# Two MLP layers in transposed tiles: the widths of the last two token pairs change places

## The chip, the cores and the metric

The kernel runs on one core of one Trainium2 chip. The metric is the device time of one execution in microseconds (us); lower is better. The kernel before takes 1495.45 us, the median of three runs (1495.42 to 1497.24).

## The reference

Attention without softmax (squared ReLU of the scores), then two MLP layers over the same 6016 tokens, all in float32:

```
scores = matmul(z, z.T) / S              # z: 2 x 3008 x 64
x = u * matmul(maximum(scores, 0)**2, v) # u, v: 2 x 3008 x 256
h = x @ w_in;  x = (h - tanh(h)) @ w_out             # 256 -> 2048 -> 256
x = (sigmoid(x @ w_gate) * (x @ w_val)) @ w_out2     # 256 -> 1536 -> 256
```

## The kernel before

Everything is kept transposed: features lie on the 128 partitions and tokens along the free dimension. A float32 product is made of three matmuls (L523 to L525, L630 to L635): each operand is cut in a high part that the fast float format holds (written by ScalarE) and the rest (written by VectorE), and high times high, high times low and low times high are summed in PSUM.

The attention comes first (to about 480 us) and isn't touched. Then come the two MLP layers. Each works on six *pairs* of token tiles; `PAIR_WIDTHS` (L65) holds the tokens of one tile of each pair, and `pair_width(q)` and `pair_token(q)` give the width and the first token of pair q. Pairs 0 to 5 belong to the first MLP, pairs 6 to 11 to the second, with the same six widths. A pair is worked through in *units* of two blocks of hidden features: 8 units in the first MLP, 6 in the second.

For a unit n TensorE makes the first products of a 2x2 block scheme with seven products in place of eight (`product`, L619): seven products of three matmuls in the first MLP (21), twice that in the second (42, for gate and value). They go to PSUM tile `hidden`. ScalarE and VectorE take them out (`snapshot`, L870 to L875; `combine`, L1136), apply tanh or sigmoid, subtract or multiply, and split the result in `part_hi` (ScalarE, `high`, L882) and `part_lo` (VectorE, `low`, at L1046, a helper that all splits share). With these the second products (`second`, L699 to L716) add 24 matmuls a unit to PSUM tile `acc`. The order of TensorE's work is written out by hand (L785 to L799): the first products of unit n alternate with the second products of unit n - 1. A pair has therefore 8 x (21 + 24) = 360 matmuls in the first MLP and 6 x (42 + 24) = 396 in the second. Each matmul loads its own 128 x 128 weights, in the instruction before it (engine PEld in the rows).

At the change of pairs the two widths mix for one unit: the first products have the new width, the second products still the old one. In unit 0 of a pair ScalarE writes the finished `acc` of the pair before to `x_out` (`evacuate`, L910 to L916), two tiles in one instruction for each half; in the first MLP the last of these instructions stands in unit 1 (L978 and L979). The first `second` call of the new pair waits for it:

```
                pe.wait_ge(s_lo, half_done(n, b))
                if u == 0 and b < 2:
                    ...
                        pe.wait_ge(s_evac, 2 * q - b)
```

Also during a pair, the next pair's tokens are loaded (`load_x`, L436, on SyncE's queue), combined (`sum_x`, L1094 to L1108) and split (`split_x`, L855 and L1046). `x_out` is stored by SyncE's queue (`store_pair`, L464). The last pair ends by itself: `last_highs` and `last_lows` (L723 to L737), then three evacuations and three stores of one tile and half each (L1034 to L1040, L1294, L513 to L516).

Of the kernel before, what the change touches and what calls it, by code (L numbers as in the profile page):

```python
# [61 lines left out]
    return T // TPB * SEQ + T % TPB * TOK  # L62


PAIR_WIDTHS = (512, 512, 512, 512, 496, 464)  # L65
assert len(PAIR_WIDTHS) == PAIRS and 2 * sum(PAIR_WIDTHS) == ALL and max(PAIR_WIDTHS) <= TOK


def pair_width(q):
    return PAIR_WIDTHS[q % PAIRS]  # L70


def pair_token(q):
    return 2 * sum(PAIR_WIDTHS[:q % PAIRS])

# [1263 lines left out]
```

## Time and profile before

| What | Value |
|---|---|
| median of three runs | 1495.45 us (1495.42 to 1497.24) |
| the profiled execution | 1496.93 us |
| its span, first to last instruction | 1495.1 us |
| TensorE busy | 1489.9 us, 8796 matmuls |
| weight loads (PEld) busy | 1256.0 us |
| VectorE busy | 1135.4 us |
| ScalarE busy | 949.5 us |
| DMA | 241.79 MB, mean 162 GB/s |

A matmul's busy time here is about 0.37 to 0.39 us, but the next one starts some 0.21 to 0.23 us after it: they are pipelined. So neither "busy" nor the mean duration of a matmul is its price; the price is the distance between the starts of two neighbours, which is read from the timeline or from the number of matmuls in a stretch of known length.

### The profile page before, as it was taken

To read this page: it belongs to the slowest core of one execution; us is meant where nothing else is said; L and a number is where in the kernel's file an instruction comes from. 1 tells how busy PE (TensorE), PEld (TensorE's weight loads), DVE (VectorE), ACT (ScalarE), POOL (GpSimd) and SP (SyncE) were. 2 spreads that over 40 slices of the span, in tenths; PEclk is the share of its full clock that TensorE was granted. 3 is DMA by queue.
4 is the path that set the end of the run, shared out by engine and by line. 5 is a ranking of instruction groups with operands and counts; after the bars stand their busy time and mean duration, and the time that the engine had idled before them with its cause. 6 is when DMAs were issued, how large, how long until landed. Compare 5 with 4: busy or idle time off the path is not lost.

```text
span 1495.1 us, 21893 instructions
## 1 busy us (share of the span) xinstructions
PE 1489.9 (100%) x8796; PEld 1256.0 (84%) x8796; DVE 1135.4 (76%) x1416; ACT 949.5 (64%) x1285; POOL 0.5 (0%) x5
## 2 busy tenths in 40 slices
PE   9999999999999999999999999999999999999999
PEld 8888888888888888888888888888888888888888
DVE  8999988999987787777676777666666676666656
ACT  8677767777766666666666666655556555555554
POOL 0000000000000000000000000000000000000000
PEclk9999999999999999999999999999999999999999
DMA  4444422254434345453535456453636454554452
GB/s 141 139 162 151 152 81 86 89 213 159 159 121 172 116 154 186 155 196 131 211 138 186 155 177 234 172 191 127 246 127 218 156 199 173 190 186 185 151 194 89
DMA packets 37365, 241.79 MB, mean 162 GB/s; under 512 B 3600, under 2 KB 8720, under 8 KB 23952
## 3 DMA queue, kind: packets, MB, share of 16 engines
q1 hardware_dynamic: 37120, 240.16, 44.1%
q8 instruction: 69, 1.13, 0.3%
q14 instruction: 32, 0.26, 0.1%
q10 hardware_dynamic: 144, 0.24, 0.0%
HBM read 196.21 MB, written 44.17 MB: 161 GB/s over the span
## 4 chain that ended last, share of the span: by engine, by line
PE 100%; ACT 0%; DVE 0%; issue 0%; DVEq 0%
PE acc L563 25%; PE hidden L632 13%; PE hidden L635 13%; PE hidden L630 13%; PE acc L524 10%; PE acc L525 10%; PE acc L523 10%; PE hidden L550 6%; PE acc L729 0%; PE acc L743 0%; PE acc L736 0%; DVE x_out L1294 0%; ACT part_hi L935 0%; ACT h L932 0%; DVE part_lo L1165 0%
## 5 line engine op out<-in xcount | busy, mean ns | idle before, releaser
L1046 DVE TENSOR_TENSOR part_lo<-h,part_hi 128x1024 fp32r<-128x1024 f32 (+5 forms) x317 | 375.2, 1184 | 82.3 <-ACT part_hi L882 49.9
L874 ACT ACTIVATE snap<-hidden 128x512 f32<-128x512 f32 (+2 forms) x360 | 211.8, 588 | 249.3 <-PE hidden L635 249.0
L632 PE MATMUL hidden<-region 128*128 128x512 f32 (+2 forms) x840 | 323.6, 385 | 0.0
L630 PE MATMUL hidden<-region 128*128 128x512 f32 (+2 forms) x840 | 323.6, 385 | 0.0
L635 PE MATMUL hidden<-region 128*128 128x512 f32 (+2 forms) x840 | 323.5, 385 | 0.0
L563 PE MATMUL acc<-part_hi,region 64*128 64x512 f32 (+1 forms) x2256 | 286.1, 383 | 0.7 <-ACT part_hi L935 0.7
L1136 DVE TENSOR_TENSOR h<-hidden,snap 128x512 f32<-128x512 f32 (+2 forms) x252 | 170.7, 678 | 142.5 <-ACT snap L874 115.7
L525 PE MATMUL acc<-part_hi,region 128*128 128x512 f32 (+2 forms) x664 | 256.1, 386 | 0.0
L524 PE MATMUL acc<-part_lo,region 128*128 128x512 f32 (+2 forms) x664 | 256.0, 386 | 0.0
L523 PE MATMUL acc<-part_hi,region 128*128 128x512 f32 (+2 forms) x664 | 255.9, 385 | 0.0
L563 PEld LDWEIGHTS acc<-part_hi,region 64*128 64x128 f32 x2256 | 216.1, 184 | 39.4 <-issue 1.1
L953 ACT ACTIVATE part_hi<-h 128x1024 fp32r<-128x1024 f32 (+1 forms) x143 | 149.3, 1044 | 129.8 <-PE acc L563 129.0
L882 ACT ACTIVATE part_hi<-h 128x1024 fp32r<-128x1024 f32 (+2 forms) x164 | 170.7, 1041 | 79.9 <-DVE h L1274 42.5
L630 PEld LDWEIGHTS hidden<-region 128*128 128x128 f32 x840 | 157.7, 188 | 30.5 <-issue 0.3
L632 PEld LDWEIGHTS hidden<-region 128*128 128x128 f32 x840 | 157.7, 188 | 29.4
L635 PEld LDWEIGHTS hidden<-region 128*128 128x128 f32 x840 | 157.7, 188 | 29.3
L1188 DVE TENSOR_TENSOR h<-h 128x1024 f32<-128x1024 f32 (+1 forms) x143 | 170.9, 1195 | 0.0
L563 PE MATMUL acc<-part_lo,region 64*128 64x512 f32 (+1 forms) x1128 | 156.4, 383 | 0.0
L523 PEld LDWEIGHTS acc<-part_hi,region 128*128 128x128 f32 x664 | 124.6, 188 | 23.8
L524 PEld LDWEIGHTS acc<-part_lo,region 128*128 128x128 f32 x664 | 124.7, 188 | 23.4
L525 PEld LDWEIGHTS acc<-part_hi,region 128*128 128x128 f32 x664 | 124.7, 188 | 23.4
L941 ACT ACTIVATE h<-hidden 128x1024 f32<-128x1024 f32 (+1 forms) x143 | 142.0, 993 | 0.8 <-PE hidden L550 0.2
(68 smaller groups left out, 1149.9 us busy)
## 6 DMA issues: line engine op xcount, KB each, us to landing
region<-ready SPq DMA_DIRECT2D x33, 2304.0 KB, 8.8
region<-ready SPq DMA_DIRECT2D x51, 1408.0 KB, 6.1
ready<-region SPq DMA_DIRECT2D x6, 2304.0 KB, 7.4
ready<-region SPq DMA_DIRECT2D x8, 1408.0 KB, 6.0
xs<-x_out SPq DMA_DIRECT2D x18, 512.0 KB, 6.0
x_in<-xs SPq DMA_DIRECT2D x16, 512.0 KB, 8.1
snap<-vP SPq DMA_DIRECT2D x24, 256.0 KB, 2.7
u_in<-uT SPq DMA_DIRECT2D x10, 512.0 KB, 5.2
```

The lines of the kernel that those rows point to most:

```text
L523: pe.matmul(dst, w_hi, x_hi, start=start, stop=False, skip_group_check=True)
L524: pe.matmul(dst, w_hi, x_lo, start=False, stop=False, skip_group_check=True)
L525: return pe.matmul(dst, w_lo, x_hi, start=False, stop=stop, skip_group_check=True)
L563: last = pe.matmul(acc[:, 2 * r + d, 0:w], v[ROWS[r], 2 * p + c, half], a[ROWS[r], 2 * (s % 2) + c, 0:w], start=start, stop=False, skip_gr ...
L630: pe.matmul(dst, weights[0], x[0], start=i < 3, stop=False, skip_group_check=True)
L632: pe.matmul(dst, weights[0], x[1], start=False, stop=False, skip_group_check=True)
L635: pe.matmul(dst, weights[1], x[0], start=False, stop=True, skip_group_check=True).then_inc(s_prod[group_of(n, s) % 2], 1)
L874: act.activation(snap[:, g % 2, i, 0:w], hidden[:, CHAIN[g % 2], 0:w], ACT.Copy).then_inc(s_snap, 1)
L882: act.activation(part_hi[:, b, 0:w], h[:, n % 2, b, 0:w], ACT.Copy).then_inc(s_hi, 1)
L1046: return ve.tensor_tensor(dst, whole, hi.bitcast(F32), ALU.subtract)
L1136: ve.tensor_tensor(dst, hidden[:, (BANK2, BANK7, BANK7)[i], 0:w], snap[:, g % 2, (0, 2, 1)[i], 0:w], ALU.add).then_inc(s_add, 1)
L1188: ve.tensor_tensor(full[:, k, :, 0:w], first[:, k, :, 0:w], first[:, k, :, 0:w], ALU.mult).then_inc(s_full, 1)
```

## The change

The last two entries of `PAIR_WIDTHS` change places. Pair 4 of the first MLP and pair 10, its counterpart in the second, hold 464 tokens a tile in place of 496; pairs 5 and 11 hold 496 in place of 464. The number of instructions, their order and the number of columns in all stay the same; the pairs' first tokens, their loads and their stores follow from the widths.

```diff
-PAIR_WIDTHS = (512, 512, 512, 512, 496, 464)
+PAIR_WIDTHS = (512, 512, 512, 512, 464, 496)
```

## Rows read from the trace of the kernel before

**Rows 1.** The page, parts 1 and 2: busy time by engine, TensorE's granted clock.

```profile
PE 1489.9 (100%) x8796; PEld 1256.0 (84%) x8796; DVE 1135.4 (76%) x1416; ACT 949.5 (64%) x1285; POOL 0.5 (0%) x5
PEclk9999999999999999999999999999999999999999
```

**Rows 2.** Stretches of one width, TensorE: us, busy (matmuls), clock, DMA share, GB/s.

```profile
820.00:880.00 60.00, 60.00 (x270) 1.00 0.41 147
1340.00:1400.00 60.00, 60.00 (x274) 1.00 0.43 163
1425.00:1485.00 60.00, 60.00 (x289) 1.00 0.36 135
1000.00:1060.00 60.00, 60.00 (x267) 1.00 0.46 176
```

**Rows 3.** Timeline of TensorE, pair 4 after its unit 0: start, us, engine, line.

```profile
819.74 0.39 PE L523 MATMUL acc<-part_hi,region 128*128 128x496 f32 x1
...
821.08 0.39 PE L523 MATMUL acc<-part_hi,region 128*128 128x496 f32 x1
```

**Rows 4.** The same, in pair 10.

```profile
1343.76 0.38 PE L524 MATMUL acc<-part_lo,region 128*128 128x496 f32 x1
...
1345.08 0.38 PE L632 MATMUL hidden<-region 128*128 128x496 f32 x1
```

**Rows 5.** The same, where pair 4 comes to its first `second` call.

```profile
814.14 0.39 PE L635 MATMUL hidden<-region 128*128 128x496 f32 x1
814.37 0.39 PE L523 MATMUL acc<-part_hi,region 128*128 128x496 f32 x1
```

**Rows 6.** The weight loads there.

```profile
813.93 0.19 PEld L635 LDWEIGHTS hidden<-region 128*128 128x128 f32 x1
814.20 0.19 PEld L523 LDWEIGHTS acc<-part_hi,region 128*128 128x128 f32 x1
```

**Rows 7.** ScalarE's evacuation that this call waits for, in pair 4 and pair 5.

```profile
813.07 1.02 ACT L915 ACTIVATE x_out<-acc 128x1024 f32<-128x1024 f32 x1
...
893.09 0.99 ACT L915 ACTIVATE x_out<-acc 128x992 f32<-128x992 f32 x1
```

**Rows 8.** Timeline, change from pair 10 to 11: 496 between 464, early and late.

```profile
1406.12 0.38 PE L523 MATMUL acc<-part_hi,region 128*128 128x496 f32 x1
...
1407.44 0.37 PE L630 MATMUL hidden<-region 128*128 128x464 f32 x1
...
1413.18 0.38 PE L523 MATMUL acc<-part_hi,region 128*128 128x496 f32 x1
...
1414.52 0.38 PE L630 MATMUL hidden<-region 128*128 128x464 f32 x1
```

**Rows 9.** Timeline, change from pair 5 to 6: 464 between 512.

```profile
960.38 0.37 PE L523 MATMUL acc<-part_hi,region 128*128 128x464 f32 x1
...
961.64 0.39 PE L630 MATMUL hidden<-region 128*128 128x512 f32 x1
```

**Rows 10.** VectorE's split of the next pair's tokens in pair 5: min/median/max ns.

```profile
L1046 DVE TENSOR_TENSOR region<-x_in,region x7: 682/682/682, 921.3 to 949.5; 128x512 fp32r<-128x512 f32 x7
```

**Rows 11.** Timeline of the tail.

```profile
1490.92 0.19 PEld L736 LDWEIGHTS acc<-part_lo,region 128*128 128x128 f32 x1
...
1491.51 0.37 PE L736 MATMUL acc<-part_lo,region 128*128 128x464 f32 x1
1491.99 0.64 DVE L1294 COPY x_out<-acc 128x464 f32<-128x464 f32 x1 [1.11 <-PE acc L736]
1492.65 0.33 SPq L516 DMA_DIRECT2D yT<-x_out  x1
```

**Rows 12.** Groups by shape: VectorE's combine at 496 and at 464.

```profile
L1136 DVE TENSOR_TENSOR h<-hidden,snap 128x496 f32<-128x496 f32 x42 | 28.2, 672 | 24.8 <-ACT snap L874 20.4 <-PE hidden L635 4.4
L1136 DVE TENSOR_TENSOR h<-hidden,snap 128x464 f32<-128x464 f32 x42 | 26.8, 638 | 26.3 <-ACT snap L874 21.9 <-PE hidden L635 4.4
```

**Rows 13.** DMA issues: one of the last stores, KB, median us to landing.

```profile
yT<-x_out SPq DMA_DIRECT2D x3, 232.0 KB, 2.1
```

## The prediction, made before the changed kernel was run

> **What bounds the kernel now.** I read the page first. TensorE is busy for 1489.9 of 1495.1 us at the full granted clock of 2.4 GHz in every slice, and no other engine is over 76% [rows 1]. The chain of waits shows the same: it runs through TensorE's lines for 100% of the span. The list of waits has ScalarE waiting for TensorE and VectorE for ScalarE, and next to nothing the other way. So the time is a sum of distances between the starts of neighbouring matmuls, and I looked at that distance for each width. A 60 us window also counts the one or two matmuls that were still running at its start (one lasts some 0.38 us), so 60 us hold about 1.7 fewer starts than the count. The stretch at 512 tokens then gives 60 / 265.3 = 226 ns, the one at 464 gives 60 / 287.3 = 209 ns. The two stretches at 496 tokens differ: pair 4 gives 60 / 268.3 = 223.6 ns, pair 10 gives 60 / 272.3 = 220.3 ns [rows 2]. The timeline gives it exactly: six starts take 1.34 us in pair 4, which is 223.3 ns each [rows 3], and 1.32 us in pair 10, which is 220.0 ns each [rows 4]. The same shape, the same weights' size, the same clock, and yet two rhythms, 3.3 ns apart, each held for its whole pair. I call 220.0 ns the even rhythm and 223.3 ns the uneven one.
>
> **Where the uneven rhythm starts.** Pair 4 began in the even rhythm too. At its first second product a matmul follows 0.23 us after its neighbour in place of 0.22 [rows 5], and its weight load starts 814.20 - 813.93 = 0.27 us after the load before it in place of 0.22 [rows 6]. It had to wait for the evacuation of pair 3, which ends at 813.07 + 1.02 = 814.09 us [rows 7]. The direct loss is 10 to 20 ns. But from there on the pair stays at 223.3 ns to its end: 60 us later it's still there [rows 2, 3]. I found no place where a run of 496-wide matmuls went back to the even rhythm by itself.
>
> **What the change adds and removes on TensorE.** The matmuls are the same 8796 and the columns are the same in sum: 360 matmuls of each width in the first MLP and 396 of each in the second. If each width has one price, the change is worth nothing there. So the question is the rhythm in which the 496-wide matmuls run once they come after 464-wide ones rather than 512-wide ones. The trace shows this at the change from pair 10 to pair 11, where 464 and 496 alternate for a unit. The first block of six at 496 takes 1407.44 - 1406.12 = 1.32 us, the even rhythm. A few microseconds later such a block takes 1414.52 - 1413.18 = 1.34 us, the uneven one [rows 8]. Nothing else changed but that more 464-wide matmuls had run. A 464-wide matmul takes 209 ns where columns alone would scale 220.0 by 464/496 to 206, and its weight load takes 0.19 us: it runs close to the load, with less room to bring a shifted load back. My reading is that the 464-wide stretch leaves the loads shifted, and that the 496-wide pair takes this over.
>
> - First MLP: pair 5 is the 496-wide one after the change. Of the 360 before, 33 ran at 220.0 (those ahead of the wait at 814.1: 21 in the mixed unit and 12 behind it) and the rest at 223.3. After: all 360 at 223.3. That is 33 x 3.3 ns = +0.11 us.
> - Second MLP: pair 11 is the 496-wide one. Before, 378 of the 396 ran at 220.0 (all but three blocks of six late in the mixed unit, of which [rows 8] show one). After: all at 223.3, +378 x 3.3 ns = +1.25 us. If the even rhythm holds instead, this term is 0; that is its lower bound.
> - 464-wide matmuls, now after 512-wide ones: a block of six between 512-wide ones takes 961.64 - 960.38 = 1.26 us, 210 ns each [rows 9], and a long stretch 209 [rows 2]. I take 209 as before: 0. From below: 206 by columns would give back 756 x 3 ns = 2.3 us, which no row shows for any block. From above: 212, if 464 had an uneven rhythm of its own, +2.3 us; no row shows that for a long stretch either.
>
> **Covers that could be gone.** In pairs 4 and 10 the evacuation of the pair before is 1024 elements wide beside 464-wide matmuls; the nearest row is pair 5's with 992 elements, 0.99 against 1.02 us [rows 7]. The wait at L709 could be 0.03 us longer, once in each MLP: 0 to +0.1 us, I take 0. In pairs 4 and 10 units of 464 carry the loading, combining and splitting of 496-wide tokens. Pair 5 carried 512-wide ones beside 464 without moving TensorE from 209 ns: seven splits of 682 ns [rows 2, 10]. So that costs 0. The x loads and the weights' loads keep their place in SyncE's queue; in pairs 4 and 10 their units are shorter by 5%, as they were in pairs 5 and 11, with DMA busy for 0.36 to 0.48 of the time [rows 2]: 0.
>
> **The tail.** What follows the last matmul is now for 496 tokens. VectorE's copy of 0.64 us [rows 11] grows by the step between 464 and 496 of such an operation, 672 - 638 = 0.03 us [rows 12]; the last matmul's own end by 32 columns, 0.01 us; the last store of 232 KB takes 2.1 us to land [rows 13] and grows to 248 KB: between 0 and 2.1 x 16/232 = 0.14 us. I take +0.1 us in all, bounds 0.04 to 0.2. The last unit's chain (VectorE's product, ScalarE's high part, VectorE's low part) reaches TensorE just in time: its weight load of L736 starts at 1490.92 [rows 11], about when it would anyway. After the change this chain's four operations grow by some 0.03 us each, 0.12, and the 22 matmuls beside it by 11 to 14 ns each, 0.24 to 0.31 us. TensorE stays the later one, and the cover gets better.
>
> **The sum.** 0.11 + 1.25 + 0 + 0.1 = +1.46 us. On the profiled execution, 1496.93 us (span 1495.1 us and 1.8 around it), this gives 1498.4. The median of the runs, 1495.45, is 1.5 us below the profiled execution; on it the sum gives 1496.9. The three runs themselves lie at 1495.42, 1495.45 and 1497.24. It may be that pair 4 wasn't in the uneven rhythm in the two shorter ones; 327 matmuls x 3.3 ns are 1.1 us. No profile of them shows it.
>
> The Trainium skill speaks against this forecast. Its page "TensorE: Matmul & The Clock Gate", section "Back-to-back issue gap", gives the distance of two matmuls as N / 2.4 GHz + 2.5 ns when warm, for the matmul alone, and says that in a stream with weight loads both set it. By the formula alone the price depends on N only, 209.2 ns at 496, and the swap would be worth nothing on TensorE. The rows agree with its slope between 512 and even 496 (226 to 220.0 ns, 16 columns), and with neither its constant nor the second price at 496; the measured distances decide.
>
> **The rivals.**
> 1. *Price by width alone.* The 496-wide matmuls of pair 11 keep 220.0 ns, because it was the late evacuation and not the neighbourhood that shifted them, and 512 or the wait of a new pair sets the rhythm back. For it: pair 4's shift did begin at a wait [rows 5, 6]. After the change the evacuation in pair 11 is narrower and early. Against it: the 1.34 us block in [rows 8], with no such wait in its unit's first half. Then only the tail and the small term of the first MLP are left, +0.1 to +0.2: 1495.6.
> 2. *Both pairs even.* As rival 1, and pair 5 is even too: 327 x 3.3 ns = 1.08 us are gained, less 0.1 for the tail: 1494.5. Against it: in the first MLP the evacuation ends later in the unit than in the second, and the pair begins in 464's rhythm.
> 3. *The timed runs before had both 496 pairs even,* and after both are uneven: 756 x 3.3 ns + 0.1 = +2.6: 1498.0. For it: the 1.8 us between the timed runs; against it: the profile.
> 4. *Slower beyond the measurement.* The 464-wide pairs enter straight from 512 and lock into an uneven rhythm of their own, at 212 ns in place of 209. The place is the first unit of pairs 4 and 10; it decides once their long stretches are above 211 ns. The price is 756 x 3.3 ns = 2.5 us on top of the 1.46: +4.0, 1499.4. For it: a single 464-wide block between 512-wide ones was already at 210 [rows 9]. Against it: the long 464 stretches of both MLPs, entered from two different rhythms, settled at the same 209 ns.
>
> **How the numbers follow.** The forecast (both 496 pairs uneven) 0.55, rival 1 0.17, rival 2 0.06, rival 3 0.12, rival 4 0.05, anything else 0.05. The range holds the forecast, rivals 1 and 3, and their bounds of a few tenths: 1495.0 to 1498.5. About 0.2% (3.0 us) is what a measurement of this kernel can tell from no change. The forecast and rivals 1 and 2 lie within it, rival 3 nearly at its edge at 1498.4, rival 4 beyond. Slower by over 0.2%: rival 4, a quarter of rival 3 and of the rest, 0.09. Faster by over 0.2% needs 3 us less of a gapless TensorE: 0.01. Same: 0.90.
>
> **What would show it.** In the trace of after, pair 11's long stretch at 496: six starts in 1.34 us (forecast) or 1.32 (rival 1). Pair 5's: the same question (rival 2). The long 464 stretches at 209 (or 212, rival 4), TensorE without a gap at L709, and from the last L736 matmul to the end of the span about 3.7 us, where before has 1495.1 - 1491.5 = 3.6 [rows 11]. The prediction is wrong if a 496-wide pair after a 464-wide one runs evenly, or if the two rhythms turn out to be set by something that differs from one execution to the next.

## The result

The changed kernel takes 1498.45 us (median of 19 runs, 1497.63 to 1499.01). The kernel before, on the same chip, takes 1495.42 us (19 runs, 1494.64 to 1497.37). The medians lie 3.0 us apart; the ratio is 1.0018 with a 95% interval of 1.0012 to 1.0024, which is 1.8 to 3.6 us. That is clear of the noise, and it lies on the 0.2% (3.0 us) that the prediction drew as its line for "same", which the interval spans. The prediction was +1.5 us, 1496.9, with a range up to 1498.5: the measured change is twice the forecast one, and the time lies 0.05 us inside the range.

The profiled execution of after took 1497.91 us, its span is 1496.1 us. The page, parts 1 and 2, beside [rows 1]:

```profile
PE 1490.8 (100%) x8796; PEld 1270.6 (85%) x8796; DVE 1135.4 (76%) x1416; ACT 949.6 (63%) x1285; POOL 0.5 (0%) x5
PEclk9999999999999999999999999999999999999999
```

Nothing new waits. TensorE is still without a gap and at full clock; VectorE and ScalarE did the same work. The 14.6 us more of weight loads lie in the attention (419.6 us busy against 404.8); in the two MLPs it is 851 us in both traces. Where the time went shows in the long stretches of one width, the answer to [rows 2]. In order: pair 4 (464 tokens), pair 5 (496), pair 10 (464), pair 11 (496), and 512 for comparison; the columns are the stretch, TensorE's busy time and its matmuls, the clock, the DMA share and GB/s:

```profile
815.00:875.00 60.00, 60.00 (x288) 1.00 0.48 169
890.00:950.00 60.00, 60.00 (x271) 1.00 0.56 203
1335.00:1395.00 60.00, 60.00 (x289) 1.00 0.50 186
1420.00:1480.00 60.00, 60.00 (x270) 1.00 0.36 136
1000.00:1060.00 60.00, 60.00 (x266) 1.00 0.46 176
```

Both 496-wide pairs have 270 or 271 matmuls in 60 us, where before's pair 10 had 274 [rows 2]. The timeline of TensorE in pair 11 has six starts in 1426.87 - 1425.54 = 1.33 to 1.34 us, as pair 4 of before [rows 3] and unlike its pair 10 [rows 4]. It is so from its first six products on, 1400.40 - 1399.06 = 1.34 us, straight behind the long stretch of 464:

```profile
1399.06 0.39 PE L630 MATMUL hidden<-region 128*128 128x496 f32 x1
...
1400.40 0.39 PE L630 MATMUL hidden<-region 128*128 128x496 f32 x1
...
1425.54 0.38 PE L523 MATMUL acc<-part_hi,region 128*128 128x496 f32 x1
...
1426.87 0.39 PE L630 MATMUL hidden<-region 128*128 128x496 f32 x1
```

The trace keeps the starts to the ns, and they show what "even" and "uneven" are. In the even rhythm every distance at 496 is 220 ns. In pair 11 of after the distances go round 227, 222, 221, 223, and their mean is 223.3; pair 4 of before does the same, and pair 5 of after stays between 222 and 225 with the same mean.

The first and the last matmul of the two MLPs in after:

```profile
479.37 0.50 PE L630 MATMUL hidden<-region 128*128 128x512 f32 x1
...
1492.31 0.39 PE L736 MATMUL acc<-part_lo,region 128*128 128x496 f32 x1
```

So the MLP part, from the first start to the last, takes 1012.9 us. Before has its last start at 1491.51 [rows 11] and its first here:

```profile
480.31 0.50 PE L630 MATMUL hidden<-region 128*128 128x512 f32 x1
```

That makes 1011.2 us. The change is +1.75 us, and the tail behind the last start grew from 3.61 to 3.77 us. The span grew by 1.0 us only, because the attention part, which isn't touched, happened to be 0.94 us shorter in this execution. The spans of two single executions can't be compared to a microsecond; their MLP parts can.

### The profile page after: what moved, and what is told of

It reads as the page before. It is cut to its first block, busy times and chain, and to the rows that moved or that the text cites. A ratio compares the mean times of both kernels' runs of the same rounds, so it can differ in the third digit from the quotient of the medians.

```text
span 1496.1 us, 21893 instructions
## 1 busy us (share of the span) xinstructions
PE 1490.8 (100%) x8796; PEld 1270.6 (85%) x8796; DVE 1135.4 (76%) x1416; ACT 949.6 (63%) x1285; POOL 0.5 (0%) x5
## 4 chain that ended last, share of the span: by engine, by line
PE 100%; ACT 0%; DVE 0%; issue 0%; DVEq 0%
PE acc L563 25%; PE hidden L630 13%; PE hidden L635 13%; PE hidden L632 13%; PE acc L523 10%; PE acc L525 10%; PE acc L524 10%; PE hidden L550 6%; PE acc L729 0%; PE acc L743 0%; PE acc L736 0%; DVE x_out L1294 0%; ACT part_hi L935 0%; ACT h L932 0%; DVE part_lo L1165 0%
## 5 line engine op out<-in xcount | busy, mean ns | idle before, releaser
L635 PE MATMUL hidden<-region 128*128 128x512 f32 (+2 forms) x840 | 323.8, 386 | 0.0
L523 PE MATMUL acc<-part_hi,region 128*128 128x512 f32 (+2 forms) x664 | 256.0, 386 | 0.0
L563 PEld LDWEIGHTS acc<-part_hi,region 64*128 64x128 f32 x2256 | 224.3, 184 | 30.7 <-issue 1.1
L635 PEld LDWEIGHTS hidden<-region 128*128 128x128 f32 x840 | 157.7, 188 | 29.9
L523 PEld LDWEIGHTS acc<-part_hi,region 128*128 128x128 f32 x664 | 124.6, 188 | 23.8
```

The costliest lines, as they stand in the source:

```text
L523: pe.matmul(dst, w_hi, x_hi, start=start, stop=False, skip_group_check=True)
L563: last = pe.matmul(acc[:, 2 * r + d, 0:w], v[ROWS[r], 2 * p + c, half], a[ROWS[r], 2 * (s % 2) + c, 0:w], start=start, stop=False, skip_gr ...
L635: pe.matmul(dst, weights[1], x[0], start=False, stop=True, skip_group_check=True).then_inc(s_prod[group_of(n, s) % 2], 1)
```

## The experiments

### The kernel before once more

Edit: none.

> The kernel before once more, unchanged, for a second trace of it. The trace on record had pair 4 (496 tokens) at 223.3 ns a matmul and pair 10 at 220.0, and its execution took 1496.9 us where the median of all timed runs of before is 1495.4. Theory: the rhythm of pair 4 differs from one execution to the next (it hangs on an evacuation that ends within some 0.05 us of TensorE's need), so a new trace may show pair 4 at 220.0, and then its MLP part is about 327 x 3.3 ns = 1.1 us shorter than the 1011.2 us (first to last MLP matmul) of the trace before. Rival: pair 4 is always uneven; then the MLP part is 1011.2 +- 0.1 us again, and the spread of the timed runs comes from the attention part or from outside.

Median 1495.77 us, ratio 1.0001 (0.9993 to 1.0010); its profiled execution took 1495.4. Pair 4 and pair 10:

```profile
820.00:880.00 60.00, 60.00 (x274) 1.00 0.39 145
1340.00:1400.00 60.00, 60.00 (x274) 1.00 0.42 158
```

Pair 4 is even here: 274 where the trace on record had 270 [rows 2]. The MLP part is 1010.2 us. TensorE's matmuls counted off in pairs (360 to a pair in the first MLP, 396 in the second, in the order in which they ran; so a few of the pair ahead stand at the start of each), in us:

| pair | before | before again | after |
|---|---|---|---|
| 4 | 80.20 | 79.20 | 76.08 |
| 5 | 75.74 | 75.74 | 80.24 |
| 10 | 87.08 | 87.08 | 83.28 |
| 11 | 82.76 | 82.76 | 88.03 |
| these four | 325.8 | 324.8 | 327.6 |
| all other pairs | 685.4 | 685.4 | 685.3 |

The two traces of the same kernel differ in one pair alone, by 1.0 us. The rhythm of pair 4 is loose: it comes out one way or the other. The trace that the prediction rested on was that of one of the slower executions.

### One MLP at a time

Each of the two kernels has its own widths for the first and the second MLP:

```diff
-    return PAIR_WIDTHS[q % PAIRS]
+    return LAYER_WIDTHS[q // PAIRS][q % PAIRS]
```

`pair_token` follows, and the load of x for pairs 10 and 11 waits for all of the first MLP's stores, since the pairs of the two MLPs no longer cover the same tokens.

> Only the first MLP's last two pairs change places (464, 496); the second keeps 496, 464. Theory of rhythms as predicted: pair 5 (496 after 464) uneven at 223.3 ns, pair 10 (496 after 512) even at 220.0. Against the trace of before +0.1 us in the MLP part; against the typical timed run, if pair 4 is mostly even in those, up to +1.2 us: 1495.5 to 1496.7. Rival, price by width alone: 1495.4, pair 5 at 220.0.

> Only the second MLP's last two pairs change places. Theory of rhythms: pair 11 (496 after 464) at 223.3 ns where pair 10 had 220.0, 378 x 3.3 ns = +1.25 us, and +0.15 us in the tail: 1496.8. With e2's part this should add up to the whole change (+3.0 us by the timed medians). Rival, price by width alone: only the tail, 1495.6, pair 11 at 220.0.

With the first MLP alone: 1496.47 us, ratio 1.0002 (0.9993 to 1.0011). With the second alone: 1497.62 us, ratio 1.0013 (1.0004 to 1.0022). The kernel before had 1495.81, timed beside them. Stretches of the first (pair 5, pair 10), then of the second (pair 4, pair 11):

```profile
890.00:950.00 60.00, 60.00 (x270) 1.00 0.56 204
1340.00:1400.00 60.00, 60.00 (x274) 1.00 0.43 162
```

```profile
820.00:880.00 60.00, 60.00 (x270) 1.00 0.40 145
...
1420.00:1480.00 60.00, 60.00 (x271) 1.00 0.35 136
```

In each MLP it is the swap that makes its 496-wide pair uneven: pair 5 in the first kernel, pair 11 in the second. Pair 10, left after a 512-wide pair, stays even. Pair 4 of the second kernel, also left after 512, was uneven in this trace, the loose one again. By the medians the parts are +0.7 and +1.8 us, 2.5 together where both at once had +3.0; the traces' MLP parts, 1011.3 and 1012.6 us, are 1.1 and 2.4 above 1010.2, and of the 2.4, 1.0 is pair 4's.

### 512 between 464 and 496, and 496 not in the last place

```diff
-PAIR_WIDTHS = (512, 512, 512, 512, 496, 464)
+PAIR_WIDTHS = (512, 512, 512, 464, 512, 496)
```

> Widths 512, 512, 512, 464, 512, 496 in both MLPs: the last pair is as wide as in the changed kernel, with the same tail, but it follows a 512 pair and not the 464 one. Theory, the neighbour sets the rhythm: pair 11 is even at 220.0 ns, 1.25 us less than the changed kernel. Pair 5 follows a 512 pair as pair 4 did in before, with the same late evacuation of 1024 elements, so it is uneven if that is what tips it (trace of before) or even if not. Sum: 1498.45 - 1.25 = 1497.2 with pair 5 uneven, 1496.1 with pair 5 even. Rival, the last place in the order is what makes 496 uneven: 1498.4, both at 223.3.

```diff
-PAIR_WIDTHS = (512, 512, 512, 512, 496, 464)
+PAIR_WIDTHS = (512, 512, 512, 464, 496, 512)
```

> Widths 512, 512, 512, 464, 496, 512: 496 directly after 464 as in the change, but no longer in the last place. Theory, the narrower neighbour ahead sets the uneven rhythm: pairs 4 and 10 at 223.3 ns, 512 at 226.7, MLP part as in the changed kernel, 1012.9 us. Rival, the last place does it: both at 220.0, 1010.4.

With 512 between, pairs 5 and 11 (496) give:

```profile
890.00:950.00 60.00, 60.00 (x274) 1.00 0.58 211
1420.00:1480.00 60.00, 60.00 (x274) 1.00 0.35 134
```

With 464 directly ahead but not last, pairs 4 and 10 (496) give:

```profile
815.00:875.00 60.00, 60.00 (x270) 1.00 0.40 145
...
1340.00:1400.00 60.00, 60.00 (x270) 1.00 0.44 165
```

Both 496 pairs even in the first, MLP part 1010.3 us; both uneven in the second, 1012.6 us. So the neighbour ahead decides and not the last place. With 464 ahead, 496 was uneven in eight of eight pairs (5 and 11 in the two traces of after, one each with one MLP at a time, 4 and 10 here). Transfers aren't what differs: pairs 5 and 11 had DMA shares of 0.58 and 0.35 with 512 between and 0.56 and 0.36 in after. The last pair, the tail and the number of matmuls of each width are the same in the first of these kernels and in after, which is 2.6 us longer in the MLP part. The medians are 1496.74 (ratio 1.0006, 0.9997 to 1.0015) and 1497.92 us (1.0007, 0.9998 to 1.0016); with intervals of 1.4 us to either side, and on two chips, they don't tell the two apart; the traces do.

### The changed kernel once more

> The changed kernel once more, unchanged, for a second trace. Theory: both 496 pairs (5 and 11) uneven again at 223.3 ns in every execution, since their 464 neighbour is always there; MLP part 1012.6 to 1013.0 us. Its pair 4 (464) ran at 210.0 ns in the first trace and at 209.0 in the trace with only the first MLP swapped, so it may show either. Rival: the rhythm of 496 after 464 is as loose as that of before's pair 4, and one of the two is even here (-1.1 or -1.3 us).

Median 1497.45 us, ratio 1.0007 (0.9998 to 1.0016), on a chip where before took 1496.64: +0.8 us where the first comparison had +3.0. The MLP part is 1012.6 us. Pairs 4, 5 and 11:

```profile
815.00:875.00 60.00, 60.00 (x289) 1.00 0.46 167
890.00:950.00 60.00, 60.00 (x271) 1.00 0.56 205
1420.00:1480.00 60.00, 60.00 (x270) 1.00 0.35 134
```

Both 496-wide pairs are uneven again. Pair 4 (464) ran at 209.0 ns here and at 210.0 in the first trace of after; that is the 0.3 us between 75.74 and 76.08, and all that differs between the two MLP parts. What made before slower on this chip wasn't seen in a trace: its pair 4 may have been uneven more often, or the attention part longer.

### What tips pair 4 of before: three tries at the evacuation

In the two traces of before the same thing happens at the first second product of pair 4. The weight load of L523 starts 0.27 us after the one ahead. In before that is [rows 6]; before again, weight loads:

```profile
813.40 0.19 PEld L635 LDWEIGHTS hidden<-region 128*128 128x128 f32 x1
813.67 0.19 PEld L523 LDWEIGHTS acc<-part_hi,region 128*128 128x128 f32 x1
813.84 0.19 PEld L524 LDWEIGHTS acc<-part_lo,region 128*128 128x128 f32 x1
```

The same shift, 271 ns in both by the trace, and then one pair stays uneven and the other is even from the seventh matmul on. So the late load can't be the whole cause; it may be what makes the outcome loose. First try, the evacuation ahead of the snapshot:

```diff
                 if n > 1:
-                    snapshot(n, 0, 0)
                     if u == 1 and q > 0:
                         evacuate(q - 1, 0)
+                    snapshot(n, 0, 0)
```

> Widths as before (496, 464). In the first MLP the evacuation that the first second product waits for is put ahead of unit 1's first snapshot, some 0.5 us earlier. The same shift of a weight load (0.27 us in place of 0.22) stood in two traces of before; in one pair 4 stayed uneven (223.3 ns), in the other it went back to 220.0. Theory: the late evacuation is what tips it; without it no weight load comes late and pair 4 is even in every execution: pair 4 at 220.0, MLP part 1010.2 us, and the upper half of the timed runs of before goes, median about 0.5 us lower, 1495.3. Rival: the rhythm is tipped by something else (a store's or load's traffic, 512 beside 496); then pair 4 is uneven in some traces still and the timed runs spread as before.

It failed as an experiment: 1498.02 us, ratio 1.0013 (1.0005 to 1.0022). TensorE's weight loads now wait for the snapshot, as the list of waits says (waiter, releaser, us in total, times, longest):

```profile
PEld hidden L630 <- ACT snap L874: 3.1, 6, 0.6
```

That is some 0.4 us in each of five pairs. Pair 4 was uneven behind this wait, with no late load of L523: so it can also be tipped where a weight load is held elsewhere. Second try, tile 0 evacuated before tile 1, both behind the snapshot:

```diff
-                        pe.wait_ge(s_evac, 2 * q - b)
+                        pe.wait_ge(s_evac, 2 * q - (1 - b if la == 0 else b))
...
                     if u == 1 and q > 0:
                         evacuate(q - 1, 0)
-                    high(n - 1, 1)
-                    snapshot(n, 0, 1)
+                        evacuate(q - 1, 1)
+                        snapshot(n, 0, 1)
+                        high(n - 1, 1)
+                    else:
+                        high(n - 1, 1)
+                        snapshot(n, 0, 1)
...
-                if u == 0 and q > 0:
-                    evacuate(q - 1, 1)
```

> Widths as before (496, 464). In the first MLP tile 0 of acc is evacuated first and tile 1 after it, both in unit 1 behind the first snapshot, and the two waits of the second products are exchanged to match. The evacuation that the first second product waits for then ends about 0.7 us sooner, ahead of need, without moving the first snapshot (which is what the other try did, and it stalled TensorE for 0.4 us a pair). The part that may stall now is the second snapshot, 0.1 to 0.5 us later. Theory, the late evacuation makes pair 4's rhythm loose: no weight load of L523 is late, pair 4 at 220.0 in the trace, MLP part 1010.2 us if nothing else waits. Rival, the late evacuation has nothing to do with it: pair 4 uneven or even regardless of that load.

Median 1496.48 us, ratio 0.9998 (0.9989 to 1.0007), MLP part 1011.3. It didn't do what it was meant to. ScalarE:

```profile
812.11 0.58 ACT L874 ACTIVATE snap<-hidden 128x496 f32<-128x496 f32 x1 [0.90 <-PE hidden L635]
812.59 1.94 ACT L915 ACTIVATE x_out<-acc 128x1024 f32<-128x1024 f32 x2
```

The snapshot now waits 0.90 us for TensorE, and the evacuation behind it ends where it ended before. The load was late by the same 0.27 us, and pair 4 was uneven. Third try, tile 0 in two halves, the first in that idle time (`evacuate_part`, new, writes one half; the wait and the rest of the order are as in the second try):

```diff
+                    if u == 1 and q > 0:
+                        evacuate_part(q - 1, 0)
                     snapshot(n, 0, 0)
                     if u == 1 and q > 0:
-                        evacuate(q - 1, 0)
+                        evacuate_part(q - 1, 1)
+                        evacuate(q - 1, 1)
...
```

> Widths as before (496, 464). The run with the exchanged order did not move the end of the awaited evacuation: the snapshot ahead of it waits for TensorE, so it ended 37 ns before the wait again, and pair 4 was uneven. Here tile 0's evacuation is cut in two: the first half runs in ScalarE's idle 0.9 us ahead of the snapshot, the second half behind it, so that it ends about 0.4 us sooner, ahead of the need. The order of the tiles and their waits are exchanged as in that run. Theory: no weight load of L523 is held (220 to 227 ns after the one before in place of 237 and 271), the wait's instruction runs ahead of its load as in the second MLP, pair 4 is even (220.0) in the trace and in all timed runs: MLP part 1010.1 us, median 1495.3 or a little less, narrow. Rival, the loose rhythm has another cause: pair 4 uneven, MLP part 1011.2, 1496.4.

Weight loads at the same place (its lines are one higher, L636 is L635 of before), and pair 4's stretch:

```profile
813.38 0.19 PEld L636 LDWEIGHTS hidden<-region 128*128 128x128 f32 x1
813.60 0.19 PEld L524 LDWEIGHTS acc<-part_hi,region 128*128 128x128 f32 x1
813.82 0.19 PEld L525 LDWEIGHTS acc<-part_lo,region 128*128 128x128 f32 x1
```

```profile
820.00:880.00 60.00, 60.00 (x274) 1.00 0.40 145
```

No load is held, 0.22 us each, and pair 4 runs at 220.0 ns from its first product to its last. The MLP part is 1010.4 us; pair 5 (464) ran at 210.0 ns in place of 209 and took 0.3 us more than in before. The median, 1495.60 us, isn't different from before's 1495.31, timed beside it (ratio 0.9999, 0.9990 to 1.0008). The timed runs didn't get narrower either, as was expected of an always even pair 4: 1494.46 to 1496.16 us, where before had 1494.82 to 1496.59.

Taken together, over all traces with a 496-wide pair behind a 512-wide one: where the evacuation ended just ahead of the wait, it was uneven in three (before, the second MLP alone, the exchanged order) and even in two (before again, 512 between). Where no load was held, it was even in eight of eight (pair 10 in six traces, pair 11 with 512 between, pair 4 with the halves). The first try, where another load was held, was uneven. This isn't proof that the held load is the cause. The five were held alike, 270 or 271 ns, and came out both ways; seven of the eight stand in the second MLP, where no load is held but the order of the work is another too; and in the first MLP there is one pair without a held load, which could be even by luck, as two of the five were.

### Other widths

```diff
-PAIR_WIDTHS = (512, 512, 512, 512, 496, 464)
+PAIR_WIDTHS = (512, 512, 512, 512, 480, 480)
```

> Widths 512 x4, 480, 480. In the traces 512 takes 226.7 ns and even 496 takes 220.0, which is (N + 32) / 2.4 ns; 464 would be 206.7 by that but takes 209, near the 188 ns of its weight load. Theory: only a width whose own distance falls below about 209 ns leaves the loads shifted; 480 stays above, at 213.3, and both pairs run evenly. The MLP part is then that of before with both 496 pairs even (1010.2 us) less 756 x 2.3 ns = 1008.5 us, 1493.8 in all by the timed runs. Rival: every width under 512 can be tipped, by about 3.3 ns: 480 at 216.7 in both MLPs, 1512 x 3.3 ns = 5.0 us more, 1498.8.

```diff
-PAIR_WIDTHS = (512, 512, 512, 512, 496, 464)
+PAIR_WIDTHS = (512, 512, 512, 512, 472, 488)
```

> Widths 512 x4, 472, 488: narrower first and wider last, as in the change, but the narrow one stays just over the distance that its weight loads allow: 210.0 ns by (N + 32) / 2.4. Theory of the threshold: 472 at 210.0, 488 even at 216.7 though it follows the narrower pair, MLP part 1008.5 us, 1494.0. Rival, any narrower neighbour tips the wider pair: 488 at 220.0 in pairs 5 and 11, 756 x 3.3 ns = +2.5 us, 1496.5.

```diff
-PAIR_WIDTHS = (512, 512, 512, 512, 496, 464)
+PAIR_WIDTHS = (502, 502, 502, 502, 500, 500)
```

> Widths 502 x4, 500, 500: no wide pair at all. By (N + 32) / 2.4 the distances are 222.5 and 221.7 ns and the MLP part is as with 480, 480: 1008.5 us, tail 0.07 us longer, 1493.9. Rival: where the late evacuation tips a pair that has no 512-wide matmuls to come back on, all six pairs of the first MLP, or of both, stay uneven: about 3.3 ns on up to 4536 matmuls, up to +15 us; pair 4's first blocks decide.

Medians 1498.02 (ratio 1.0012, 1.0003 to 1.0021), 1498.63 (1.0017, 1.0008 to 1.0026) and 1512.46 us (1.0107, 1.0092 to 1.0123); MLP parts 1013.4, 1013.7 and 1027.3 us. The stretches of 480 (pairs 4 and 11), then of 472 and 488 (pairs 4 and 5), then of 502 in pairs 0, 1 and 6:

```profile
815.00:875.00 60.00, 60.00 (x279) 1.00 0.47 170
1420.00:1480.00 60.00, 60.00 (x278) 1.00 0.41 151
```

```profile
815.00:875.00 60.00, 60.00 (x283) 1.00 0.48 173
890.00:950.00 60.00, 60.00 (x275) 1.00 0.58 209
```

```profile
490.00:550.00 60.00, 60.00 (x270) 1.00 0.42 152
590.00:650.00 60.00, 60.00 (x259) 1.00 0.40 145
1000.00:1060.00 60.00, 60.00 (x270) 1.00 0.44 165
```

The theory of a threshold at 464's weight load falls. By the starts in the traces 480 runs at 216.7 ns, 472 at 213.3 and 488 at 220.0, each 3.3 ns above (N + 32) / 2.4, and 480 does so straight behind 512, before any load is held. So "3.3 ns more" doesn't need a narrower neighbour at these widths; only for 496 did the neighbour decide. The step is the same everywhere: all mean distances in the long stretches but the 208.9 ns of 464 are whole multiples of 3.33 ns (210.0, 213.3, 216.7, 220.0, 223.3, 226.7, 233.3).

The kernel with 502 shows a change of rhythm inside one width. Its pair 0 ran at 223.3 ns, (N + 32) / 2.4 and 0.8 more, and so did pair 1 up to its first second product. There ScalarE's evacuation ended at 567.23 us and the weight load came 0.24 us after the one ahead in place of 0.22:

```profile
567.11 0.19 PEld L635 LDWEIGHTS hidden<-region 128*128 128x128 f32 x1
567.35 0.19 PEld L523 LDWEIGHTS acc<-part_hi,region 128*128 128x128 f32 x1
567.56 0.19 PEld L524 LDWEIGHTS acc<-part_lo,region 128*128 128x128 f32 x1
```

From that product on the distance is 233.3 ns, 10.8 above the formula, through pairs 1 to 3. In the second MLP, where no load is held, the long stretches of 502 stayed at 223.3. The 500-wide pairs had 223.3 ns (pair 4) and 226.7 (5, 10 and 11) for 221.7. In all these traces 512 has its price by the formula, 226.7, in the long stretches, and 496 has only behind 512.

## Why the prediction came out as it did

**The bound** was read rightly: a gapless TensorE, and a price per matmul that must be read from start to start. Nothing else moved.

**The number** was half right, and it is partly luck that the range held it. The sum gave +1.5 us, the medians say 3.0, and 1498.45 lies 0.05 us inside a range that reached that far for the sake of rival 3.

**The signs of being wrong.** The prediction named two. The first, an even 496-wide pair behind a 464-wide one, never came, in eight of eight pairs. The second, rhythms that are set by something that differs from one execution to the next, did come, though not in the changed pairs: pair 4 of before was uneven in one trace and even in the other, with the same kernel.

**The second MLP**, +1.25 us: right. Pair 11 is uneven in all three traces with 464 ahead of it and even in the one with 512 ahead. Pairs 10 and 11 together went from 169.8 to 171.3 us, +1.5. Some of the 0.2 left is in the mixed unit, which the prediction had not counted. A block of six 512-wide matmuls between 464-wide ones can take 806.65 - 805.26 = 1.39 us in after where the one ahead took 1.36. Pair 10 has three such blocks of six. Pair 4 has the one shown here, and its next six 512-wide ones, ahead of six more, took 1.39 us too:

```profile
803.27 0.39 PE L523 MATMUL acc<-part_hi,region 128*128 128x512 f32 x1
...
804.63 0.37 PE L630 MATMUL hidden<-region 128*128 128x464 f32 x1
...
805.26 0.40 PE L523 MATMUL acc<-part_hi,region 128*128 128x512 f32 x1
...
806.65 0.37 PE L630 MATMUL hidden<-region 128*128 128x464 f32 x1
```

**The first MLP**, +0.11 us: right against the first trace of before, mis-sized against the median. This is the step that failed; between an even pair 4 and pair 5 of after the runs show +1.0 us in its place. The term took pair 4 as uneven because one trace had it so, and then put the sum on a median that lay 1.5 us below that very execution. The prediction noticed both and gave it to rival 3, "the timed runs before had both 496 pairs even", with a chance of 0.12 and 1498.0 us. The repeated trace of before, with its execution at 1495.4, is that rival: pair 4 even. From it to after the MLP part grows by 2.7 us: 1.0 (496 in pair 5 against pair 4) + 1.5 (pairs 10 and 11) + 0.3 (464 at 210.0 ns) - 0.1 elsewhere. With 0.15 of tail that is 2.9 of the 3.0 measured. How many of the 19 timed runs had pair 4 even, or 464 at 210.0 ns, isn't known; that these two traces stand for the medians is argued, not shown. A trace whose own time lies in the slower part of the runs is a warning that its rhythm isn't theirs.

**464 at 209 ns**, taken as 0: true in nine of ten 464-wide pairs traced with 512 ahead, and 0.3 us in the tenth, pair 4 of the first trace of after. Its distances alternate between 205 and 215 ns there, the others' go between 207 and 210. Rival 4, 212 ns for both, did not happen.

**The covers** at nothing: right; the list of waits has no new entry for TensorE. The held load of pair 4 came 0.31 us after the one ahead where before had 0.27, that of pair 5 0.26 where before had 0.29. One reading was off without effect: the DMA share was put at 0.36 to 0.48, but pair 5 of before has 0.57 and pair 5 of after 0.56:

```profile
900.00:955.00 55.00, 55.00 (x265) 1.00 0.57 212
```

**The tail**, +0.1: 0.16 by the spans.

**Where the uneven rhythm starts**: half right. The held weight load goes with it behind 512: all eight pairs without one were even, and 502 left its 223.3 ns just there. But it doesn't decide: the same 0.27 us came out both ways, and in two pairs the rhythm went back by itself within seven matmuls, which the prediction had found nowhere. Behind 464 no held load is needed: pair 11 of after is uneven from its first product on, and its first second product's load came 0.22 us after the one ahead.

**The reason given for 464's part**, that it runs close to its weight load, isn't supported: 472, 480 and 488 have more room and are 3.3 ns above (N + 32) / 2.4 too. That the 496-wide pair takes over what stands ahead of it is supported, by its first six products above.

**Rival 1**, price by width alone, is out by the two orders with 512 between and ahead. The formula of the Trainium skill's page "TensorE: Matmul & The Clock Gate", section "Back-to-back issue gap", is of that kind. Here 496 had 220.0 and 223.3 ns and 502 had 223.3 and 233.3, so no formula of N alone fits these traces.

**Open**: what inside TensorE holds the two rhythms, and what decides at equal shifts. No row shows it; the held loads that came out differently were alike to 1 ns. Also open is why before and after lay 3.0 us apart on one chip and 0.8 on another.

## What to carry to other kernels

Where TensorE has no gaps, read the price of a matmul from start to start, for each stretch of one shape, and compare stretches of the same shape: a difference of 1.5% without any wait is worth as much as a wait. In this kernel the best of the orders tried kept as many tiles as possible at the full 512 and had 496 directly behind a 512; an even share of the remainder (480 and 480) cost 2 us, and no full tiles at all (502) cost 16. When a single trace is the base, see whether its own time is that of the typical run before putting a sum of a microsecond on the median.

## What was not expected of the hardware

A stream of weight loads and matmuls of one shape, at full clock and without a wait, had two steady mean distances, 220.0 and 223.3 ns at 496 columns, each kept for over 300 matmuls; behind 464 columns it was always the longer one. The means go in steps of 3.33 ns, so 16 columns fewer don't always buy 6.7 ns: 480 columns ran at 216.7. At 502 columns the second distance was 233.3 ns, and it cost 10 ns on each of some 1000 matmuls. A pair whose one weight load was held by 0.05 us took 1.0 us more over the 320 matmuls behind it in three of five traces, and next to nothing in the other two.
